# Four PSUM banks for the scores, and another order of work on the matrix engine, in a fused attention, MLP and routed-expert kernel

## The chip, the cores and the metric

The kernel runs as one program on one core of a Trainium2 chip. The metric is the device time of one execution in microseconds (us). The engines are TensorE (PE, matrix products; PEld is its weight load), VectorE (DVE), ScalarE (ACT), GpSimd (POOL) and SyncE (SP, which issues transfers). Each works through its own list of instructions in order; semaphores tie the lists together. PE writes its results into PSUM, eight banks of 512 float32 columns on 128 partitions.

## The reference

```python
# attention, per batch (4) and head (8): S = 576, D = 64
scores = q @ k.T / 8
kth    = the 32nd largest score of each row
attn   = softmax(where(scores >= kth, scores, -1e9))
x      = attn @ v                      # heads side by side: 2304 tokens x 512
# MLP: 512 -> 2048 -> 512
x = relu(x @ w_in) ** 2 @ w_out
# routed experts: 8 of 512 -> 1024 -> 512
compute = x @ w_skip > 0;  e = argmax(x @ w_gate);  g = softmax(x @ w_gate)[e]
out[compute] = x + g * (relu(x @ w1[e]) @ w2[e])
```

## The kernel before, in words

Attention runs in 72 steps (`NS`); step s takes 128 query rows of two heads (a "pair" step) or, in the middle group of eight, 64 left-over rows of four heads (a "mixed" step). Nine groups of eight steps (`GROUPS`, `PER_GROUP`) each fill 256 tokens of x; when a group is full, its MLP runs as 16 units (`FT`). A unit is `up` (12 matmuls of 256 columns) and `down` (6 matmuls of 512 columns) of the unit two places before. The engines' lists are written by one loop over t (`TIMES`). In iteration t the kernel does the scores of step t+1, the threshold and mask of t-1, the normalisation and transposes of t-2, the value product of t-3, and, from t = 10 (`FIRST`), two MLP units of an earlier group. So the MLP of group j fills PE while the attention of group j+1 goes on.

One step, by its names. `scores_half` (L1352, mixed L1358) multiplies q by one half of the keys, 288 columns for each of two heads. ACT copies each half to `s_sb` (`copy_scores`, L792). DVE pairs column i of the first half with column i of the second: `find_upper` (L1036) and `find_lower` (L1043) form the maxima and minima of all pairs, in one read from PSUM and in the other from `s_sb`. DVE then finds the 32nd largest with MAX8 and MATCH_REPLACE8 rounds (L1052, L1057, L1067, L1072), `pair_ranks` (L1083) and `find_kth` (L1090). POOL turns the result into two bias columns (`set_bounds`, L615 and L617), ACT computes a marker from them (`find_below`, L801, once for each head), POOL subtracts it (`mask`, L629), ACT exponentiates (L809), DVE inverts the sums (L1095) and POOL normalises (L623). PE transposes the probabilities (`transpose_probs`, L1377 and L1380), ACT copies them (`copy_transposed`, L816), PE multiplies by v (`values_product`, L1396), ACT copies the result twice (`copy_values`, L825 and L826) and POOL makes its low part (`split_x`, L635). In the MLP ACT does L834 and L843 and POOL L644 and L649 (`square_low`).

PSUM before: the scores' halves share banks 0 and 1, one after the other; the transposes use banks 2 to 4, the value product the rest of bank 4, `up` bank 5 and `down` banks 6 and 7. In three iterations of each group (`ENDS[j]`, +1, +2) PE also does the routing work on the finished group: `transpose_y` (L1449), `route_parts` (L1462) and `route` (L1473), in banks 2 and 3. After iteration 84 or so come the routed experts, about 150 us, which the change does not touch.

Unlike the order above, in the program PE's iteration before is: first half of the scores, value product, second half, transposes, unit, unit, routing. The rows of it stand in the next section but one.

Of the kernel before, what the change touches and what calls it, by code (L numbers as in the profile page):

```python
# [52 lines left out]
def build(nc, qT, kT, v_main, v_tail, w_in, w_out, w9, w1, w2, rows_scratch, out):  # L53
# [86 lines left out]
    with ExitStack() as ctx:  # L140
# [91 lines left out]
        def score_banks(s, half):  # L232


            at = 2 if s == 0 and half == 1 else 0
            return psum[:, at:at + 2, 0:HALF]

        pT_psum = psum_flat[:, 2 * 512:2 * 512 + PT_COLS]
        yT_psum = psum_flat[:, 2 * 512:4 * 512]
        values_psum = psum[:, 4, P:2 * P]  # L240
# [198 lines left out]
        def _(sp):  # L439
# [66 lines left out]
            for t in range(TIMES):  # L506
                for a in range(RING_A, len(LOADS_A)):
                    if FREED[a - RING_A] == t:
                        sp.wait_ge(scores_done, 2 * t + 2)
                        load_kq(a)  # L510
# [90 lines left out]
        def _(pool):  # L601
# [100 lines left out]
            for t in range(TIMES):  # L702
                slots = mlp_slots(t)
                if 0 <= t - 1 < NS:
                    set_bounds(t - 1)
# [3 lines left out]
                if 0 <= t - 3 < NS:  # L709
                    split_x(t - 3)  # L710
# [75 lines left out]
        def _(act):  # L786
            def copy_scores(s, half):
                act.wait_ge(scores_done, 2 * s + half + 1)
# [3 lines left out]
                nc.scalar.activation(s_sb[:, s % SBUFS, :, half * HALF:(half + 1) * HALF], score_banks(s, half), ACT.Copy,  # L792
# [19 lines left out]
            def copy_transposed(s):  # L812
                act.wait_ge(transposed, s + 1)
# [95 lines left out]
            copy_scores(0, 0)  # L909
            copy_scores(0, 1)  # L910
            for t in range(TIMES):
                slots = mlp_slots(t)
                if t + 1 < NS:
                    copy_scores(t + 1, 0)
                if 0 <= t - 1 < NS:
                    find_below(t - 1, 0)
                if 0 <= t - 3 < NS:
                    copy_values(t - 3)
                if t + 1 < NS:
                    copy_scores(t + 1, 1)  # L920
                if 0 <= t - 1 < NS:
                    find_below(t - 1, 1)
                for j in range(GROUPS):
                    if ENDS[j] == t:
                        copy_rows(j)
                if 0 <= t - 2 < NS:
                    copy_transposed(t - 2)
# [8 lines left out]
                for u in slots[0:1]:  # L936
                    square_high(u)
                if 0 <= t - 1 < NS:
                    exponentiate(t - 1, 1)
# [3 lines left out]
                for j in range(GROUPS):  # L943
                    if ENDS[j] == t:
                        copy_yT(j)
                    if ENDS[j] + 1 == t and j < GROUPS - 1:
                        copy_parts(j)
                    if ENDS[j] + 2 == t and j < GROUPS - 1:
                        copy_logits(j)
                if t == ENDS[GROUPS - 2] + 3:  # L950
# [76 lines left out]
        def _(dve):  # L1027
            v = nc.vector

            def find_upper(s):  # L1030


                dve.wait_ge(scores_copied, 2 * s + 2)

                wait(dve, upper_step, 14 * (s - 1))
                v.scalar_tensor_tensor(out=upper[:, s % 2, :, :], in0=score_banks(s, 1), scalar=SCALE,  # L1036
                                       in1=s_sb[:, s % SBUFS, :, 0:HALF], op0=ALU.mult, op1=ALU.max).then_inc(upper_set, 1)

            def find_lower(s):
# [3 lines left out]
                v.scalar_tensor_tensor(out=lower[:, s % 2, :, :], in0=score_banks(s, 1), scalar=SCALE,  # L1043
                                       in1=s_sb[:, s % SBUFS, :, 0:HALF], op0=ALU.mult, op1=ALU.min).then_inc(lower_set, 1)
# [289 lines left out]
        def _(pe):  # L1334
            t_ = nc.tensor

            def scores_half(s, half):
                kind, _, _, _, r, a = STEPS[s]
                if half == 0:
                    for x in range(a, a + (1 if kind == "pair" else 2)):  # L1340
                        pe.wait_ge(kq_loaded[x % RING_A], KQ_COUNT[x])

                if s > 0:
                    pe.wait_ge(scores_copied, 2 * s + half)
                if half == 0:
                    wait(pe, lower_set, s)
                banks = score_banks(s, half)
# [360 lines left out]
```

## Time and profile before

| | |
|---|---|
| median of 3 runs | 923.28 us (922.73 to 923.67) |
| the profiled execution: span from first to last instruction | 920.5 us |
| PE, PEld busy | 96%, 78% |
| DVE, ACT, POOL busy | 89%, 71%, 71% |
| mean granted TensorE clock | 0.985 of full |

The profiled execution has no time of its own beside the span; the runs around it are 2.2 to 3.2 us longer than the span, which is what lies outside the first and last instruction. A busy share counts an engine as busy while any of its instructions runs, and neighbouring instructions overlap at their ends. So the length of a stage is best read as the distance from its first start to the next stage's first start.

### The profile page before, as it was taken

To read this page: it belongs to the slowest core of one execution; us is meant where nothing else is said; L and a number is where in the kernel's file an instruction comes from. 1 tells how busy PE (TensorE), PEld (TensorE's weight loads), DVE (VectorE), ACT (ScalarE), POOL (GpSimd) and SP (SyncE) were. 2 spreads that over 40 slices of the span, in tenths; PEclk is the share of its full clock that TensorE was granted. 3 is DMA by queue.
4 is the path that set the end of the run, shared out by engine and by line. 5 is a ranking of instruction groups with operands and counts; after the bars stand their busy time and mean duration, and the time that the engine had idled before them with its cause. 6 is when DMAs were issued, how large, how long until landed. Compare 5 with 4: busy or idle time off the path is not lost.

```text
span 920.5 us, 21085 instructions
## 1 busy us (share of the span) xinstructions
PE 885.1 (96%) x6684; PEld 719.2 (78%) x6684; DVE 819.2 (89%) x2584; ACT 658.5 (72%) x1297; POOL 656.6 (71%) x884
## 2 busy tenths in 40 slices
PE   4799899999999999999999999999999999999997
PEld 2677687888888788888788887888878886788886
DVE  6999999999999999999999999999991064888887
ACT  3777787777777778777777777877775322788886
POOL 2999998878887787787888778778787452444432
PEclk7799999999999999999999999999999999999999
DMA  9962533566344658866535455433533675764990
GB/s 332 364 242 95 173 125 124 166 203 193 120 166 142 212 181 280 239 188 229 170 130 169 138 186 171 169 125 125 189 125 114 242 243 208 273 226 154 335 334 23
DMA packets 69750, 175.40 MB, mean 191 GB/s; under 512 B 21298, under 2 KB 26418, under 8 KB 65280
## 3 DMA queue, kind: packets, MB, share of 16 engines
q1 hardware_dynamic: 67568, 168.77, 54.2%
q0 software_dynamic: 1840, 5.06, 1.7%
q8 instruction: 56, 0.92, 0.4%
q14 instruction: 62, 0.51, 0.2%
q10 hardware_dynamic: 224, 0.15, 0.1%
HBM read 154.19 MB, written 21.27 MB: 191 GB/s over the span
## 4 chain that ended last, share of the span: by engine, by line
PE 84%; DVE 11%; POOL 2%; issue 1%; ACT 1%; DMA 0%; DVEq 0%; SPq 0%; POOLq 0%
PE psum L1352 8%; PE psum L1417 7%; PE psum L1418 7%; PE psum L1419 7%; PE psum L1377 7%; PE psum L1434 7%; PE psum L1435 7%; PE psum L1396 7%; PE psum L1436 7%; DVE top L1052 3%; DVE upper L1057 3%; PE psum L1650 2%; PE psum L1619 2%; PE psum L1624 2%; PE psum L1655 2%; PE psum L1658 2%
## 5 line engine op out<-in xcount | busy, mean ns | idle before, releaser
L1052 DVE MAX8 top<-upper 128x8 f32<-128x288 f32 x576 | 238.8, 446 | 0.0
L629 POOL TENSOR_TENSOR s_sb<-s_sb,below 128x576 f32<-128x576 f32 x144 | 203.3, 1434 | 1.5 <-ACT below L801 1.5
L1057 DVE MATCH_REPLACE8 upper<-top,upper 128x288 f32<-128x288 f32 x432 | 187.6, 441 | 0.0
L1417 PE MATMUL psum<-x_high,w_in_high 128*128 128x256 f32 x576 | 168.3, 292 | 1.6 <-POOL x_low L635 1.1
L1418 PE MATMUL psum<-x_low,w_in_high 128*128 128x256 f32 x576 | 161.8, 281 | 0.0
L1419 PE MATMUL psum<-x_high,w_in_low 128*128 128x256 f32 x576 | 161.2, 280 | 0.0
L792 ACT ACTIVATE s_sb<-psum 128x576 f32<-128x576 f32 x144 | 93.8, 651 | 93.7 <-PE psum L1352 84.2
L644 POOL TENSOR_TENSOR square<-relu 128x256 f32<-128x256 f32 x144 | 89.7, 623 | 81.7 <-ACT relu L834 80.9
L649 POOL TENSOR_TENSOR g_low<-square,g_high 128x256 fp32r<-128x256 f32 x144 | 108.4, 753 | 30.3 <-POOL square L644 23.2
L1352 PE MATMUL psum<-k_sb,q_sb 64*128 64x288 f32 x512 | 100.1, 469 | 21.7 <-DVE lower L1043 19.1
L801 ACT ACTIVATE below<-s_sb,steep_kth 128x576 f32<-128x576 f32 x144 | 110.8, 770 | 9.2 <-POOL neg_max L617 8.4
L1067 DVE MAX8 top<-lower 128x8 f32<-128x288 f32 x288 | 115.3, 441 | 0.0
L1434 PE MATMUL psum<-w_ring,g_high 128*128 128x512 f32 x288 | 114.5, 398 | 0.0
L1435 PE MATMUL psum<-w_ring,g_high 128*128 128x512 f32 x288 | 113.5, 394 | 0.0
L1436 PE MATMUL psum<-w_ring,g_low 128*128 128x512 f32 x288 | 113.2, 393 | 0.0
L1417 PEld LDWEIGHTS psum<-x_high,w_in_high 128*128 128x128 f32 x576 | 108.5, 188 | 6.0 <-POOL x_low L635 1.3
L1418 PEld LDWEIGHTS psum<-x_low,w_in_high 128*128 128x128 f32 x576 | 108.7, 189 | 3.2
L809 ACT ACTIVATE s_sb<-s_sb,neg_max 128x576 f32<-128x576 f32 x144 | 110.9, 770 | 0.0
L834 ACT ACTIVATE relu<-psum 128x256 f32<-128x256 f32 x144 | 55.5, 385 | 76.1 <-PE psum L1419 75.0
L1419 PEld LDWEIGHTS psum<-x_high,w_in_low 128*128 128x128 f32 x576 | 108.6, 189 | 0.0
L623 POOL TENSOR_SCALAR s_sb<-s_sb,sums 128x576 f32<-128x576 f32 x144 | 106.3, 749 | 0.0
L1377 PEld LDWEIGHTS psum<-ident,s_sb 128*128 128x128 f32 x576 | 62.1, 142 | 34.0 <-issue 30.2
(213 smaller groups left out, 1848.0 us busy)
## 6 DMA issues: line engine op xcount, KB each, us to landing
w_ring<-w_split SPq DMA_DIRECT2D x144, 512.0 KB, 4.5
weights<-w SPq DMA_DIRECT2D x32, 1024.0 KB, 7.1
v_sb<-v_main SPq DMA_DIRECT2D x48, 256.0 KB, 2.5
w_split<-w_ring SPq DMA_DIRECT2D x16, 512.0 KB, 4.3
k_sb<-kT SPq DMA_DIRECT2D x32, 144.0 KB, 4.5
k_sb<-kT SPq DMA_DIRECT2D x32, 128.0 KB, 4.3
weights<-w_out SPq DMA_DIRECT2D x1, 4096.0 KB, 13.5
weights<-w_in SPq DMA_DIRECT2D x1, 4096.0 KB, 21.1
```

Source lines behind the costliest of these rows:

```text
L629: nc.gpsimd.tensor_tensor(s_sb[:, s % SBUFS, n, 0:S], s_sb[:, s % SBUFS, n, 0:S], below[:, n, :], ALU.subtract).then_inc(masked, 1)
L1052: v.max(top[:, s % 2, n, 8 * r:8 * r + 8], upper[:, s % 2, n, :]).then_inc(upper_step, 1)
L1057: v.match_replace(upper[:, s % 2, n, :], top[:, s % 2, n, 8 * r:8 * r + 8], upper[:, s % 2, n, :], LOWEST).then_inc(upper_step, 1)
L1067: v.max(top[:, s % 2, n, at:at + 8], lower[:, s % 2, n, :]).then_inc(lower_step, 1)
L1352: last = t_.matmul(banks[:, n, :], q_sb[own, a % RING_A, r * P:(r + 1) * P], k_sb[own, a % RING_A, cols], start=True, stop=True)
L1377: t_.transpose(psum[:, 2 + n, k * P:(k + 1) * P], tiles[:, at:at + P], ident[:, :])
L1417: t_.matmul(dst, wh, x_high[:, j % 2, k, :], start=k == 0, stop=False)
L1418: t_.matmul(dst, wh, x_low[:, j % 2, k, :], start=False, stop=False)
L1419: last = t_.matmul(dst, wl, x_high[:, j % 2, k, :], start=False, stop=k == KC - 1)
L1434: t_.matmul(psum[:, 6 + c, :], gh, wh, start=f == 0, stop=False)
L1435: t_.matmul(psum[:, 6 + c, :], gh, wl, start=False, stop=False)
L1436: last = t_.matmul(psum[:, 6 + c, :], gl, wh, start=False, stop=f == FT - 1)
```

## The change

The two halves of the scores get banks of their own: the first half banks 0 and 1, the second banks 2 and 3. The second half shares its banks with the transposes and the routing work, so each of these waits for the other's copy. The scores of a step are now done in one piece and copied by ACT with one instruction over four banks (128x1152). DVE's pair passes read the first half from PSUM and the second from `s_sb`. PE's iteration becomes: scores, unit, transposes of t-2, unit, routing, value product of t-2 (no longer t-3). ACT and POOL follow that order: `copy_values` and `split_x` come first in the iteration, both `find_below` come before the scores' copy, and `copy_transposed` comes after the first exponential. The first unit of a group may start its first chunks of k before the last low part of x is there.

On PE, an iteration in the middle of the program (`U` and `D` of the text are the L1417 to L1419 and the L1434 to L1436 matmuls), before:

```order
L1352 MATMUL psum<-k_sb,q_sb 128x288 x2
L1396 MATMUL psum<-pT_sb,v_sb 64x128 x8
L1396 MATMUL psum<-pT_sb,v_last 64x128 x2
L1352 MATMUL psum<-k_sb,q_sb 128x288 x2
L1377 MATMUL psum<-ident,s_sb 128x128 x8
L1380 MATMUL psum<-ident,s_sb 128x128
L1417 MATMUL psum<-x_high,w_in_high 128x256
```

The same place after, from the value product on (L1411 is the value product, L1350 the scores, L1437 to L1439 and L1454 to L1456 a unit, L1394 and L1395 the transposes; the dots leave out repeats inside a unit):

```order
L1411 MATMUL psum<-pT_sb,v_sb 64x128 x8
L1411 MATMUL psum<-pT_sb,v_last 64x128 x2
L1350 MATMUL psum<-k_sb,q_sb 128x288 x4
L1437 MATMUL psum<-x_high,w_in_high 128x256
...
L1456 MATMUL psum<-w_ring,g_low 128x512
L1394 MATMUL psum<-ident,s_sb 128x128 x8
L1395 MATMUL psum<-ident,s_sb 128x128
L1437 MATMUL psum<-x_high,w_in_high 128x256
```

The two pieces of scores have become one, a unit stands between them and the transposes, and the value product has moved from between the scores' halves to the end of the iteration.

On ACT, one iteration before:

```order
L792 ACTIVATE s_sb<-psum 128x2x288
L801 ACTIVATE below<-s_sb,steep_kth 128x576
L825 ACTIVATE x_now<-psum 128x128
L826 ACTIVATE x_high<-psum 128x128
L792 ACTIVATE s_sb<-psum 128x2x288
L801 ACTIVATE below<-s_sb,steep_kth 128x576
L816 ACTIVATE pT_sb<-psum 128x1152
L834 ACTIVATE relu<-psum 128x256
L809 ACTIVATE s_sb,sums<-s_sb,neg_max 128x576
L843 ACTIVATE g_high<-relu 128x256
```

and after (L833 and L834 copy the values, L807 is `find_below`, L791 the scores' copy, L842 and L851 the unit's, L815 the exponential, L824 the transposes' copy):

```order
L833 ACTIVATE x_now<-psum 128x128
L834 ACTIVATE x_high<-psum 128x128
L807 ACTIVATE below<-s_sb,steep_kth 128x576 x2
L791 ACTIVATE s_sb<-psum 128x1152
L842 ACTIVATE relu<-psum 128x256
L815 ACTIVATE s_sb,sums<-s_sb,neg_max 128x576
L851 ACTIVATE g_high<-relu 128x256
L824 ACTIVATE pT_sb<-psum 128x1152
```

The scores' copy now stands behind both `find_below`, which wait for POOL's bounds of step t-1.

The diff, cut to what the prediction speaks of:

```diff
         @block.gpsimd: for t in range(TIMES):
+                if 0 <= t - 3 < NS:
+                    split_x(t - 3)
                 if 0 <= t - 1 < NS:
                     set_bounds(t - 1)
                 if 0 <= t - 2 < NS:
                     normalise(t - 2, 0)
                     normalise(t - 2, 1)
-                if 0 <= t - 3 < NS:
-                    split_x(t - 3)
...
+            def copy_scores(s):
+                act.wait_ge(scores_done, s + 2)
                 if s >= SBUFS:
                     act.wait_ge(transposed, s - SBUFS + 1)
+                nc.scalar.activation(s_sb[:, s % SBUFS, :, :].rearrange("p n (h c) -> p n h c", h=2),
+                                     psum[:, 0:4, 0:HALF].rearrange("p (h n) c -> p n h c", h=2), ACT.Copy,
+                                     scale=SCALE).then_inc(scores_copied, 1)
...
             def find_upper(s):
-                dve.wait_ge(scores_copied, 2 * s + 2)
+                dve.wait_ge(scores_copied, s + 2)
                 wait(dve, upper_step, 14 * (s - 1))
-                v.scalar_tensor_tensor(out=upper[:, s % 2, :, :], in0=score_banks(s, 1), scalar=SCALE,
-                                       in1=s_sb[:, s % SBUFS, :, 0:HALF], op0=ALU.mult, op1=ALU.max).then_inc(upper_set, 1)
+                v.scalar_tensor_tensor(out=upper[:, s % 2, :, :], in0=score_banks(0), scalar=SCALE,
+                                       in1=s_sb[:, s % SBUFS, :, HALF:S], op0=ALU.mult, op1=ALU.max).then_inc(upper_set, 1)
...
+            def scores(s):
...
+                if s > 0:
+                    pe.wait_ge(scores_copied, s + 1)
+                wait(pe, lower_set, s)
+                last = scores_half(s, 0)
...
+                wait(pe, transposed_copied, s - 3)
...
+                scores_half(s, 1).then_inc(scores_done, 1)
 
             def transpose_probs(s):
+                pe.wait_ge(scores_copied, min(s + 3, NS - 1) + 2)
                 wait(pe, transposed_copied, s)
+                wait(pe, values_copied, s)
...
             def up(u):
+                whole = KC - 1 if ORDER[j] else KC - 2
                 if f == 0:
-                    pe.wait_ge(x_low_done, PER_GROUP * (j + 1))
+                    pe.wait_ge(x_low_done, PER_GROUP * (j + 1) - (2 if ORDER[j] else 1))
...
                 for k in range(KC):
+                    if f == 0 and k == whole:
+                        pe.wait_ge(x_low_done, PER_GROUP * (j + 1))
...
             for t in range(TIMES):
                 if t + 1 < NS:
-                    scores_half(t + 1, 0)
-                if 0 <= t - 3 < NS:
-                    values_product(t - 3)
-                if t + 1 < NS:
-                    scores_half(t + 1, 1)
-                if 0 <= t - 2 < NS:
-                    transpose_probs(t - 2)
+                    scores(t + 1)
                 if 2 <= t < FIRST:
                     keep_clock(20)
+                if not slots and 0 <= t - 2 < NS:
+                    transpose_probs(t - 2)
                 for u in slots:
                     up(u)
                     down(u - DOWN_LAG)
...
+                    if u % 2 == 0 and 0 <= t - 2 < NS:
+                        transpose_probs(t - 2)
+                routing_share(t)
+                if 0 <= t - 2 < NS:
+                    values_product(t - 2)
```

`routing_share(t)` holds the calls of `transpose_y`, `route_parts` and `route` that stood at the iteration's end before. `copy_rows` moves from the start of iteration `ENDS[j]` to the end of the one before it.

## Rows read from the trace of the kernel before

**Rows 1.** The page: busy us, share of the span and instructions of each engine.

```profile
PE 885.1 (96%) x6684; PEld 719.2 (78%) x6684; DVE 819.2 (89%) x2584; ACT 658.5 (72%) x1297; POOL 656.6 (71%) x884
```

**Rows 2.** Timeline, PE, one ordinary step: start us, us, instructions merged.

```profile
244.86 0.76 PE L1352 MATMUL psum<-k_sb,q_sb 64*128 64x288 f32 x4
245.54 1.09 PE L1396 MATMUL psum<-pT_sb,v_sb 128*64 128x128 f32 x16
...
246.78 0.76 PE L1352 MATMUL psum<-k_sb,q_sb 64*128 64x288 f32 x4
247.47 1.09 PE L1377 MATMUL psum<-ident,s_sb 128*128 128x128 f32 x8
...
248.43 0.36 PE L1417 MATMUL psum<-x_high,w_in_high 128*128 128x256 f32 x1
...
249.93 0.39 PE L1434 MATMUL psum<-w_ring,g_high 128*128 128x512 f32 x1
...
252.74 0.39 PE L1434 MATMUL psum<-w_ring,g_high 128*128 128x512 f32 x1
...
254.22 0.51 PE L1352 MATMUL psum<-k_sb,q_sb 64*128 64x288 f32 x2
```

**Rows 3.** Timeline, PE: four iterations later, three of them with routing work.

```profile
263.60 0.76 PE L1352 MATMUL psum<-k_sb,q_sb 64*128 64x288 f32 x4
...
303.04 0.71 PE L1358 MATMUL psum<-k_sb,q_mixed 64*64 64x288 f32 x8
```

**Rows 4.** Timeline, DVE: ends of search 56.62, 65.95, 243.91; then one pair pass.

```profile
56.62 0.16 DVE L1090 TENSOR_REDUCE kth<-mins 128x2 f32<-128x34 f32 x1
...
65.95 0.16 DVE L1090 TENSOR_REDUCE kth<-mins 128x2 f32<-128x34 f32 x1
...
243.91 0.17 DVE L1090 TENSOR_REDUCE kth<-mins 128x2 f32<-128x34 f32 x1
...
250.30 0.75 DVE L1036 SCALAR_TENSOR_TENSOR upper<-psum,s_sb 128x576 f32<-128x576 f32 x1
```

**Rows 5.** Timeline, PE, the first scores of the program.

```profile
4.38 2.01 PE L1352 MATMUL psum<-k_sb,q_sb 64*128 64x288 f32 x8 [0.30 <-DMA k_sb<-kT]
...
10.19 1.33 PE L1352 MATMUL psum<-k_sb,q_sb 64*128 64x288 f32 x4 [0.74 <-ACT s_sb L792]
```

**Rows 6.** Timeline, ACT, in the step of rows 2.

```profile
246.90 0.28 ACT L825 ACTIVATE x_now<-psum 128x128 f32<-128x128 f32 x1
247.08 0.27 ACT L826 ACTIVATE x_high<-psum 128x128 fp32r<-128x128 f32 x1
...
248.13 0.77 ACT L801 ACTIVATE below<-s_sb,steep_kth 128x576 f32<-128x576 f32 x1
248.80 1.13 ACT L816 ACTIVATE pT_sb<-psum 128x1152 f32<-128x1152 f32 x1
```

**Rows 7.** Timeline, POOL, in the same step.

```profile
244.73 0.73 POOL L649 TENSOR_TENSOR g_low<-square,g_high 128x256 fp32r<-128x256 f32 x1
245.43 0.20 POOL L615 TENSOR_SCALAR steep_kth<-kth 128x2 f32<-128x2 f32 x1
245.59 0.19 POOL L617 TENSOR_SCALAR neg_max<-top 128x2 f32<-128x2 f32 x1
...
247.43 0.46 POOL L635 TENSOR_TENSOR x_low<-x_now,x_high 128x128 fp32r<-128x128 f32 x1 [0.20 <-ACT x_high L826]
247.85 1.43 POOL L629 TENSOR_TENSOR s_sb<-s_sb,below 128x576 f32<-128x576 f32 x1
```

**Rows 8.** Timeline, POOL, near 27 us.

```profile
25.70 2.49 POOL L657 TENSOR_TENSOR w_ring<-weights,w_ring 128x512 fp32r<-128x512 f32 x2
```

**Rows 9.** Timeline, DVE, at the same time.

```profile
27.21 1.03 DVE L1083 TENSOR_TENSOR mins<-top 128x34 f32<-128x34 f32 x1
```

**Rows 10.** Timeline, PE, after the last scores.

```profile
689.54 0.63 PE L1377 MATMUL psum<-ident,s_sb 128*128 128x128 f32 x4 [0.49 <-POOL s_sb L623]
...
716.07 0.39 PE L1417 MATMUL psum<-x_high,w_in_high 128*128 128x256 f32 x1 [1.08 <-POOL x_low L635]
```

More of the change, by code:

```diff
@@ L942, in _ @@
                     square_high(u)
-                for j in range(GROUPS):
+                for j in range(GROUPS - 1):
                     if ENDS[j] == t:
                         copy_yT(j)
-                    if ENDS[j] + 1 == t and j < GROUPS - 1:
+                    if ENDS[j] + 1 == t:
                         copy_parts(j)
-                    if ENDS[j] + 2 == t and j < GROUPS - 1:
+                    if ENDS[j] + 2 == t:
                         copy_logits(j)
+                for j in range(GROUPS):
+                    if ENDS[j] - 1 == t:
+                        copy_rows(j)
+                if t == ENDS[GROUPS - 1]:
+                    copy_yT(GROUPS - 1)
                 if t == ENDS[GROUPS - 2] + 3:
@@ L1338, in scores_half @@
                 kind, _, _, _, r, a = STEPS[s]
[L1339 to L1347, printed above, removed]
                 cols = slice(half * HALF, (half + 1) * HALF)
@@ L1351, in scores_half @@
                         own = slice(n * HD, (n + 1) * HD)
-                        last = t_.matmul(banks[:, n, :], q_sb[own, a % RING_A, r * P:(r + 1) * P],
+                        last = t_.matmul(psum[:, 2 * half + n, 0:HALF], q_sb[own, a % RING_A, r * P:(r + 1) * P],
                                          k_sb[own, a % RING_A, cols], start=True, stop=True)
@@ L1513, in _, with routing_share @@
             keep_clock(5)
-            scores_half(0, 0)
-            scores_half(0, 1)
+            def routing_share(t):
+                for j in range(GROUPS - 1):
+                    if ENDS[j] == t:
+                        transpose_y(j)
+                    if ENDS[j] + 1 == t:
+                        route_parts(j)
+                    if ENDS[j] + 2 == t:
+                        route(j)
+            scores(0)
             for t in range(TIMES):
@@ L1542, in _ @@
                     up_ahead(0, [0])
-                for j in range(GROUPS):
-                    if ENDS[j] == t:
-                        transpose_y(j)
-                    if ENDS[j] + 1 == t and j < GROUPS - 1:
-                        route_parts(j)
-                    if ENDS[j] + 2 == t and j < GROUPS - 1:
-                        route(j)
+                    transpose_y(GROUPS - 1)
                 if t == ENDS[GROUPS - 1] + 1:
```

69 lines of the change are left out of this document (33 added, 36 removed).

## The prediction

> **What bounds the kernel now.** I read the page first: PE is busy 96% of the span and DVE 89%, ACT and POOL 71% each [rows 1]. In the attention part PE and DVE are both busy without a break, so busy shares can't tell which sets the pace. The timeline can, by the distance from one step's start to the next.
>
> DVE alone: before the MLP has begun, when PE has room, its search ends come 65.95 - 56.62 = 9.33 us apart [rows 4]. That is DVE's own pace.
>
> PE alone, one ordinary step, start to start [rows 2]: scores half 0.68 (244.86 to 245.54), value product 1.24, scores half 0.69, transposes 0.96, first `up` 1.50, `down`, `up` 2.81, second `down` 1.48. The sum is 9.36, no stage among them has an idle time in the timeline, so PE works back to back, a hair slower than DVE. With routing work four steps take 303.04 - 263.60 = 39.44 [rows 3], which is 4 x 9.36 + 2.0. So a group of eight costs PE 8 x 9.36 + 2.0 = 76.9 and DVE only 8 x 9.33 = 74.6. PE sets the pace, with DVE 2.3 us per group behind it. The reader is to see that a PE step made shorter by more than some 0.3 us brings nothing more.
>
> **What PE saves in a step.** The counts of matmuls stay. What goes is one change between kinds of product. A lone half lasts 0.69, although its columns account for less: the nine transposes of 128 columns take 0.96 [rows 2], 0.107 each, so 288 columns are 0.24, and a half is two of these in each of two row groups that run side by side, 0.48. The 0.2 left is filling and emptying. Joined, a half is to cost 0.48 more, not 0.69 more: 0.69 + 0.48 = 1.17. Bounds for the joined piece: above 1.37, two lone halves; below, eight instructions took 2.01 where four took 1.33 at the low clock [rows 5], a ratio of 1.51, and 1.51 x 0.69 = 1.04 (the clock rose during the eight, so this is too low). I take 1.17, near the column count.
>
> The other changes of kind in the new order: scores to `up` is not in the trace; transposes to `up` costs the unit 1.50 against 1.42 (2.81 less a `down` of 1.39), so I take 1.50, bounds 1.42 and 1.60 (what a half loses altogether). Value product to scores 1.24 as now. `down` to value product 1.48, as `down` to scores now. `down` to transposes and routing: 1.39, and the transposes then lack part of their fill, 0.92 (0.90 to 0.96). The step becomes 1.24 + 1.17 + 1.50 + 1.39 + 0.92 + 1.50 + 1.48 = 9.20, or 0.16 less. A group becomes 8 x 9.20 + 2.0 = 75.6, 1.3 less, and PE still sets the pace, 1.0 above DVE. Over the 62 iterations that hold both attention and units (t = 10 to 71) PE saves 62 x 0.16 = 9.9. In the first nine of them, before any routing, DVE's 9.33 holds PE back, so 9 x 0.13 = 1.2 of it is not had. First term: -9.
>
> The Trainium skill weighs the same place by a rule: "Changing tiling mode (not just tile) drains the TensorE" (TensorEngine Tiling (Array Packing), Tiling Modes). Scores use 64-row tiles, values 64-column ones, all else the full array. By the rule four changes of mode in a step become three, and what is saved is one drain and no column time. With the whole 0.2 of a half as the drain the rule gives the same 9.2. The step of rows 2 shows the loss at each such change but cannot show whether scores to `up` costs as much as scores to transposes.
>
> **What the copies cost.** ACT copied two halves of 0.65; now it copies 1152 columns at once. The trace has that size: 1.13 [rows 6], which is contiguous where the new one is in four pieces. ACT's total falls by a tenth, and ACT isn't the bound. What counts is where the copy stands. Before, the second half's copy had only one L801 ahead; now both stand ahead, and they wait for POOL's bounds, which stand behind `split_x`, which waits for the value product. And the transposes now wait for the copy. That makes a loop through PE:
>
> value product ends; to ACT 0.1; `copy_values` 0.45 (246.90 to 247.35) [rows 6]; to POOL 0.08; `split_x` 0.42 (247.43 to 247.85); L615 and L617 0.35 (245.43 to 245.78) [rows 7]; to ACT 0.03; two L801 at 0.68 (248.13 to 248.80), 1.35; the copy 1.13 [rows 6]; to PE 0.05. Together 3.96 from the value product to the transposes. PE itself gets there by scores, `up`, `down`: 1.17 + 1.50 + 1.39 = 4.06. So the transposes find the copy done 0.1 us before, and the loop costs nothing; behind the waiting transposes stand the unit, routing and value product of the iteration, so any wait would lengthen the step in full. Cost taken: 0, with bounds of 0 and 0.07 per step, for a copy between 1.13 and 1.30 (two halves of 0.65). In iterations with routing PE's part of the loop grows by the same work as PE's step, so the 0.1 stays.
>
> DVE needs the copy 6.2 us after its own `find_kth` ended (243.91 + 0.17 to 250.30) [rows 4]; the way there is 0.1 + 0.35 + 0.03 + 1.35 + 1.13 = 3.0. DVE isn't kept waiting. The waits for the previous transposes' copy and for `copy_rows`, moved on ACT, are for work that ended a whole unit (2.8) earlier. SP's loads hang on the same counts as before, and the v slots are freed an iteration earlier for a product that comes nearly an iteration earlier; the lead stays over a step. No cost.
>
> **After the last scores.** There PE waits for POOL before the transposes (0.49 for the first head, about 0.2 for the second, in two steps, and half that in a third) and 1.08 for the last low part of x [rows 10]. After, a unit (2.8 us) stands ahead of the transposes and covers the first; the last value product is an iteration earlier and the first unit's leading chunks cover the second. Together 0.7 + 0.7 + 0.4 + 1.1 = 2.9, of which nothing else on PE takes the place. Second term: -3.
>
> **The sum.** 920.5 - 9 - 3 = 908.5 as a span. The runs are a median of 2.8 above the span, so 911.3 against 923.28.
>
> **Rivals.**
>
> The first: DVE's pace holds. If joined scores come near 1.04 and `up` loses nothing, PE's group falls to DVE's 74.6. The attention steps then gain (76.9 - 74.6) per group over 7.75 groups, 17.8, less the first nine steps' share of about 3, and 3 behind: about 906. For it: rows 5. Against: that ratio spans a rise of the clock. Chance 0.13.
>
> The second: half of it goes in new losses on PE. The joined scores stay nearer 1.37 less 0.1, or leaving them costs `up` 0.1 more: saved 0.06 to 0.08 a step, 5 us, plus 3: 916. Chance 0.10, and 0.05 for the end of this case in which nothing is left, 923.
>
> The third: POOL holds DVE up. L1083 took 1.03 us where it takes 0.17, and it ended with POOL's L657 (25.70 + 2.49 = 28.19 against 27.21 + 1.03 = 28.24) [rows 8, 9]. So this one DVE instruction, which reads two SBUF operands, can wait for a POOL instruction to end. The order moves POOL's work against DVE's. Where L1083 falls is between PE's scores and 5.6 us behind their end, as DVE leads or lags; POOL's masks of 1.43 [rows 7] run some 1.9 to 4.7 us behind that end while DVE is already a search further, so it can meet L644 or L649 (0.73) at the unit's end but hardly a mask. A mean hold of 0.13 us per step is hidden by PE's 75.6 against DVE's 74.6; 0.3 gives 8 x 9.63 = 77.0, no gain in the steps. Middle: 0.2, 76.2 per group, gain 5.4 + 3, 915. Chance 0.05.
> The Trainium skill has this as a rule: a DVE instruction with two SBUF inputs and a GpSimd instruction that reads SBUF lock each other out of a shared port for the whole instruction (SBUF — State Buffer, Who interferes with whom). The trace agrees, by the pair of rows at 27 us.
>
> The fourth, slower: the loop through the copy becomes the bound. It has 0.1 us to spare. The place is the transposes' wait for `scores_copied`. If the four-piece copy, or ACT's turn behind POOL, takes 0.5 longer than the rows add up to, each step is 9.20 + 0.4 = 9.60, a group 78.8, 1.9 more than before, over 7.75 groups +15, less 3 behind: 935. It decides from 0.1 and turns the sign from about 0.3. For it: five hand-overs between engines in series, none of which had slack in my sum. Against: each piece is a row. Chance 0.08.
>
> **How the numbers follow.** The forecast has 0.59, the rivals 0.13, 0.10, 0.05, 0.05 (915) and 0.08. Faster by over 0.2% (1.8 us, about what a measurement of this kernel tells from no change): 0.59 + 0.13 + 0.10 + 0.05 = 0.87, less 0.01: 0.86. Within: 0.05. Slower: 0.09. The range leaves out the slower case and "no change" above, and goes down to the DVE case: 904.5 to 919. The forecast's own range is 908 to 914, from the bounds of the joined scores (0.05 either way makes 3).
>
> **What would show it.** L1350 x4 spans about 1.17 to the first L1437; ordinary steps of 9.2 to 9.35 on PE; DVE's search ends 9.33 apart in ordinary steps; transposes (L1394) with no idle time ahead of them, from `scores_copied` above all; `pair_ranks` (L1090 now) staying at 0.17 to 0.2; no wait of 1.08 at the last group's first unit. The prediction is wrong if the transposes wait for the copy in most steps, if joined scores last over 1.3, or if DVE's step exceeds 9.5.

## The result, and the profile after

The changed kernel takes 912.55 us (median of 4 runs, 911.1 to 913.32). The kernel before took 923.16 us beside it (922.73 to 923.67). The ratio is 0.9885, with a 95% interval of 0.9871 to 0.9899. The prediction was 911.3, with a range of 904.5 to 919.

The profiled execution after has a span of 910.6 us, 9.9 less than before. In every run on record with a span listed, the time is 1.7 to 1.9 us above that run's own span. So the 2.2 to 3.2 us between the times and the 920.5 of the kernel before are not all time outside the first and last instruction: its profiled execution was itself about 1 us faster than the median. That is why the spans differ by 9.9 and the medians by 10.6. The TensorE clock is no rival here. The profiled execution before had a mean granted clock of 0.985, the one after 0.999. But other runs of the kernel before with 0.998 or more take 922.5 to 923.1 us, and those with 0.985 and 0.986 take 922.0 and 922.2.

First the page, in answer to [rows 1]:

```profile
PE 872.4 (96%) x6684; PEld 724.1 (80%) x6684; DVE 821.0 (90%) x2584; ACT 645.1 (71%) x1226; POOL 656.1 (72%) x884
```

The shares hardly changed. The gain shows in the distance between steps. (PE's matmuls and the weight loads, PEld, are listed apart.) The timeline of PE over one ordinary step answers to [rows 2] (start us, us, instructions merged; repeats inside a unit are left out):

```profile
462.85 1.24 PE L1350 MATMUL psum<-k_sb,q_sb 64*128 64x288 f32 x8
464.02 0.39 PE L1437 MATMUL psum<-x_high,w_in_high 128*128 128x256 f32 x1
...
465.56 0.39 PE L1454 MATMUL psum<-w_ring,g_high 128*128 128x512 f32 x1
...
466.95 1.03 PE L1394 MATMUL psum<-ident,s_sb 128*128 128x128 f32 x8
...
467.85 0.36 PE L1437 MATMUL psum<-x_high,w_in_high 128*128 128x256 f32 x1
...
469.36 0.39 PE L1454 MATMUL psum<-w_ring,g_high 128*128 128x512 f32 x1
...
470.86 1.09 PE L1411 MATMUL psum<-pT_sb,v_sb 128*64 128x128 f32 x16
```

From start to start: scores 1.17, `up` 1.54, `down` 1.39, transposes 0.90, `up` 1.51, `down` 1.50, and the value product 1.24 as before. That is 9.25, and 9.24 on average in ordinary steps. A group of eight, from one scores' start to that eight steps on, takes 75.7 (414.9 to 490.6). It was 76.9. In such a group PE and DVE both have no idle time now. The stretches below are one group before and one after (us; busy time of PE, PEld, DVE, ACT, POOL; then granted clock, DMA share and GB/s):

```profile
427.92:504.84 76.92, 76.92 (x605) 62.72 (x604) 75.23 (x266) 58.59 (x125) 61.44 (x89) 1.00 0.51 159
```

```profile
425.04:500.71 75.67, 75.67 (x606) 63.36 (x604) 75.67 (x267) 57.21 (x117) 61.49 (x88) 1.00 0.53 164
```

What DVE's 1.1 us beyond its own 74.6 consist of is told under the port below.

The loop through the copy, in the same steps (timeline of ACT, PE and POOL):

```profile
465.65 1.12 ACT L791 ACTIVATE s_sb<-psum 128x1152 f32<-128x1152 f32 x1
466.95 1.03 PE L1394 MATMUL psum<-ident,s_sb 128*128 128x128 f32 x8
470.86 1.09 PE L1411 MATMUL psum<-pT_sb,v_sb 128*64 128x128 f32 x16
...
472.22 0.28 ACT L833 ACTIVATE x_now<-psum 128x128 f32<-128x128 f32 x1 [1.39 <-PE psum L1411]
472.39 0.27 ACT L834 ACTIVATE x_high<-psum 128x128 fp32r<-128x128 f32 x1
472.74 0.46 POOL L633 TENSOR_TENSOR x_low<-x_now,x_high 128x128 fp32r<-128x128 f32 x1 [0.84 <-ACT x_high L834]
473.17 0.19 POOL L613 TENSOR_SCALAR steep_kth<-kth 128x2 f32<-128x2 f32 x1
473.32 0.20 POOL L615 TENSOR_SCALAR neg_max<-top 128x2 f32<-128x2 f32 x1
473.55 1.44 ACT L807 ACTIVATE below<-s_sb,steep_kth 128x576 f32<-128x576 f32 x2 [0.89 <-POOL neg_max L615]
474.90 1.11 ACT L791 ACTIVATE s_sb<-psum 128x1152 f32<-128x1152 f32 x1
```

The value product gives way to the next scores at 470.86 + 1.24 = 472.10. The copy ends at 474.90 + 1.11 = 476.01, and 0.05 more hands it to PE: 3.96. The transposes start 4.10 behind the scores' start (462.85 to 466.95). So 0.14 is to spare for the matmuls, and the loop does not set the pace here. Their weight load (PEld) has no such room: it starts at 466.82, just behind the end of the copy at 465.65 + 1.12 = 466.77.

Early on, before any routing work, DVE's 9.33 is slower than PE's 9.24. There the transposes do wait a little for the copy, which PE can afford: it is not the engine that sets the pace there. The same rows near 133 us:

```profile
134.72 1.11 ACT L791 ACTIVATE s_sb<-psum 128x1152 f32<-128x1152 f32 x1
135.88 0.86 PEld L1394 LDWEIGHTS psum<-ident,s_sb 128*128 128x128 f32 x8 [0.37 <-ACT s_sb L791]
```

Behind the last scores, PE has no idle time ahead of its transposes at 691.70, where [rows 10] had 0.49, nor ahead of the last group's first unit, where they had 1.08. But one new wait has come up at the very end of the units (timeline of ACT and PE after):

```profile
757.65 0.60 ACT L879 ACTIVATE rows<-psum 128x512 f32<-128x512 f32 x1 [3.79 <-PE psum L1456]
758.15 0.59 ACT L961 ACTIVATE ahead_xT<-psum 128x512 f32<-128x512 f32 x1
758.79 1.12 PE L1519 MATMUL psum<-weights,ahead_xT 128*128 128x512 f32 x2 [1.18 <-ACT ahead_xT L961]
```

The same place before:

```profile
767.35 0.60 ACT L954 ACTIVATE ahead_xT<-psum 128x512 f32<-128x512 f32 x1 [2.40 <-PE psum L1535]
...
768.54 1.02 PE L1499 MATMUL psum<-weights,ahead_xT 128*128 128x512 f32 x2
...
768.74 0.60 ACT L871 ACTIVATE rows<-psum 128x512 f32<-128x512 f32 x1 [0.79 <-PE psum L1436]
```

Before, ACT copied `ahead_xT` while PE was still on its last `down`. The change put `copy_rows` of the last group ahead of it in ACT's queue. That copy needs the last `down`, so `ahead_xT` now comes late. (The idle times of 2.40 and 3.79 are ACT's own.)

The 9.9 us by stretches, from the two profiled executions: up to the end of the last scores -8.3 (681.0 to 672.7). From there to the end of the last `down` -2.8 (87.7 to 84.9). Behind it +1.2 (151.8 to 153.0).

### The profile page after: what moved, and what is told of

Its sections match the earlier page's. It is cut to its first block, busy times and chain, and to the rows that moved or that the text cites. A ratio compares the mean times of both kernels' runs of the same rounds, so it can differ in the third digit from the quotient of the medians.

```text
span 910.6 us, 21039 instructions
## 1 busy us (share of the span) xinstructions
PE 872.4 (96%) x6684; PEld 724.1 (80%) x6684; DVE 821.0 (90%) x2584; ACT 645.1 (71%) x1226; POOL 656.1 (72%) x884
## 4 chain that ended last, share of the span: by engine, by line
PE 86%; DVE 12%; issue 1%; ACT 1%; DMA 0%; POOL 0%; SPq 0%; DVEq 0%
PE psum L1437 9%; PE psum L1411 8%; PE psum L1438 7%; PE psum L1439 7%; PE psum L1455 7%; PE psum L1454 7%; PE psum L1456 7%; PE psum L1350 7%; PE psum L1394 6%; DVE top L1059 3%; DVE upper L1064 3%; PE psum L1674 2%; PE psum L1643 2%; PE psum L1648 2%; PE psum L1679 2%; PE psum L1652 2%
## 5 line engine op out<-in xcount | busy, mean ns | idle before, releaser
L1437 PE MATMUL psum<-x_high,w_in_high 128*128 128x256 f32 x576 | 174.6, 303 | 0.0
L1439 PE MATMUL psum<-x_high,w_in_low 128*128 128x256 f32 x576 | 161.8, 281 | 0.0
L807 ACT ACTIVATE below<-s_sb,steep_kth 128x576 f32<-128x576 f32 x144 | 104.0, 769 | 75.4 <-POOL neg_max L615 75.4
L1437 PEld LDWEIGHTS psum<-x_high,w_in_high 128*128 128x128 f32 x576 | 108.5, 188 | 25.6 <-issue 21.9
L815 ACT ACTIVATE s_sb<-s_sb,neg_max 128x576 f32<-128x576 f32 x144 | 110.8, 769 | 9.3 <-POOL s_sb L627 2.2
L647 POOL TENSOR_TENSOR g_low<-square,g_high 128x256 fp32r<-128x256 f32 x144 | 108.6, 754 | 11.3
L1454 PE MATMUL psum<-w_ring,g_high 128*128 128x512 f32 x288 | 113.9, 396 | 0.0
L1456 PE MATMUL psum<-w_ring,g_low 128*128 128x512 f32 x288 | 113.9, 395 | 0.0
L1439 PEld LDWEIGHTS psum<-x_high,w_in_low 128*128 128x128 f32 x576 | 108.6, 189 | 0.0
L1350 PE MATMUL psum<-k_sb,q_sb 64*128 64x288 f32 x512 | 83.6, 447 | 16.1 <-DVE lower L1050 15.5
L824 ACT ACTIVATE pT_sb<-psum 128x1152 f32<-128x1152 f32 x72 | 80.4, 1116 | 8.6 <-PE psum L1395 8.6
L633 POOL TENSOR_TENSOR x_low<-x_now,x_high 128x128 fp32r<-128x128 f32 x72 | 32.8, 456 | 68.5 <-ACT x_high L834 68.5
L791 ACT ACTIVATE s_sb<-psum 128x1152 f32<-128x1152 f32 x71 | 78.9, 1112 | 3.9 <-PE psum L1350 3.9
```

Of the source, the lines that this page charges most:

```text
L815: nc.scalar.activation(tile, tile, ACT.Exp, bias=neg_max[:, s % 2, n:n + 1], accum_out=sums[:, s % 2, n:n + 1]).then_inc(exp_done, 1)
L1350: last = t_.matmul(psum[:, 2 * half + n, 0:HALF], q_sb[own, a % RING_A, r * P:(r + 1) * P], k_sb[own, a % RING_A, cols], start=True, stop= ...
L1437: t_.matmul(dst, wh, x_high[:, j % 2, k, :], start=k == 0, stop=False)
L1439: last = t_.matmul(dst, wl, x_high[:, j % 2, k, :], start=False, stop=k == KC - 1)
L1454: t_.matmul(psum[:, 6 + c, :], gh, wh, start=f == 0, stop=False)
L1456: last = t_.matmul(psum[:, 6 + c, :], gl, wh, start=False, stop=f == FT - 1)
```

## The experiments

### The copy of `ahead_xT` first

```diff
+                if t == ENDS[GROUPS - 1] - 1:
+                    act.wait_ge(ahead_transposed, 1)
+                    nc.scalar.activation(ahead_xT[:, :], psum[:, 4, :], ACT.Copy).then_inc(ahead_xT_done, 1)
                 for j in range(GROUPS):
                     if ENDS[j] - 1 == t:
                         copy_rows(j)
...
-                if t == ENDS[GROUPS - 1] - 1:
-                    act.wait_ge(ahead_transposed, 1)
-                    nc.scalar.activation(ahead_xT[:, :], psum[:, 4, :], ACT.Copy).then_inc(ahead_xT_done, 1)
```

> ScalarE copies the ahead rows (ahead_xT) before copy_rows of the last group instead of behind it. Theory: in the changed kernel PE stood idle for 1.18 us at the first up_ahead, because ahead_xT was queued on ACT behind a copy that waits for the last down product. Then the wait goes, the last down product is followed by up_ahead at once, and the time falls by 1.2 us, 912.55 to 911.4. Rival: the next thing behind it (the last rows' copies, the transposed rows, the search for the experts' places on VectorE) is late anyway and the time stays within 0.3 us.

Measured: 911.28 us (910.81 to 911.36), 1.3 less than the changed kernel's 912.55, with a ratio to before of 0.9878 (0.9861 to 0.9894). The times alone do not settle it. The kernel before took 922.58 beside this run and 923.16 beside the changed kernel, and the intervals of the two ratios overlap. The trace does: the wait is gone, and PE goes straight on at 757.65:

```profile
756.45 0.60 ACT L954 ACTIVATE ahead_xT<-psum 128x512 f32<-128x512 f32 x1 [2.40 <-PE psum L1560]
...
757.65 1.02 PE L1519 MATMUL psum<-weights,ahead_xT 128*128 128x512 f32 x2
```

From the last `down` to the end it is 151.7, as before the change (151.8), where the changed kernel has 153.0. That microsecond has its cause.

### Scores in two pieces again

```diff
             scores(0)
+            scores_rest(0)
...
+                if 0 <= t - 3 < NS:
+                    values_product(t - 3)
+                if t + 1 < NS:
+                    scores_rest(t + 1)
...
-                if 0 <= t - 2 < NS:
-                    values_product(t - 2)
```

> The value product stands between the two halves of the scores again; banks, ACT's single copy and all other orders stay as changed. Theory: what a step gained is one filling and emptying of the array between kinds of product, 0.20 us. Scores then last 0.69 + 0.69 around the value product, an ordinary step 9.24 + 0.20 = 9.44, and with 55 steps at PE's pace and the first ten at VectorE's the time rises by 10 to 12 us, to about 923, all of the gain. Rival: the gain came from the order of transposes and units (what covers what), and joining is worth little: under 3 us more.

Measured: 952.13 us (950.44 to 954.08), ratio 1.0318 (1.0298 to 1.0338). That is 40 us above the changed kernel, not some 11. The step is 9.85, within rounding of scores 0.69, values 1.24, scores 0.69, `up` 1.52, `down` 1.76, transposes 0.95, `up` 1.51, `down` 1.50. Of the 0.6 over 9.24, 0.21 is the price of two lone halves (0.69 + 0.69 against 1.17). The rest is a wait that I had not put in the sum (timeline of PE, ACT and POOL):

```profile
470.98 0.76 PE L1350 MATMUL psum<-k_sb,q_sb 64*128 64x288 f32 x4
...
471.10 0.28 ACT L833 ACTIVATE x_now<-psum 128x128 f32<-128x128 f32 x1 [1.75 <-PE psum L1413]
...
473.78 1.11 ACT L791 ACTIVATE s_sb<-psum 128x1152 f32<-128x1152 f32 x1
...
474.95 0.44 PE L1396 MATMUL psum<-ident,s_sb 128*128 128x128 f32 x2 [0.20 <-ACT s_sb L791]
```

The value product ends at 470.98, and the transposes start 3.97 later. That is the same loop again. But with only half of the scores behind the value product, PE's own way is 0.69 + 1.52 + 1.40 = 3.61, so PE waits 0.36 in every ordinary step (the 0.20 in the row is only the part that the profile puts down to this release). Only the 0.48 us of scores that joining put behind the value product keep the loop, which the prediction called harmless, from ruling the kernel. Joining saves 0.2 of scores directly, and it is also what makes the copy's place on ACT affordable.

### A longer loop

```diff
+                wait(act, pad_written, s - 1)
+                nc.scalar.activation(pad[:, :, :], ident[:, :].unsqueeze(1).to_broadcast([P, 3, P]),
+                                     ACT.Copy).then_inc(pad_written, 1)
                 nc.scalar.activation(s_sb[:, s % SBUFS, :, :].rearrange("p n (h c) -> p n h c", h=2),
```

> One more ScalarE copy of 384 columns (about 0.4 us from start to next start) stands ahead of the scores' copy in each step; its result is not used. Theory: the loop value product, values' copy, low part, bounds, two markers, scores' copy, transposes has 0.13 us to spare against PE's own way, so PE waits 0.27 us ahead of the transposes in each step, 9.24 becomes 9.5 and the time rises by 15 us (12 to 18), to 927. Rival: ACT is only 71% busy, so 0.4 us more per step costs nothing; or the loop has no slack at all, and it costs 0.4 x 60 = 24.

Measured: 933.71 us (933.26 to 934.49), ratio 1.0121 (1.0104 to 1.0138), which is 21 above the changed kernel and outside the 12 to 18 expected. The timeline of ACT and PE:

```profile
470.31 0.51 ACT L790 ACTIVATE pad<-ident 128x384 f32<-128x384 f32 x1
470.73 1.11 ACT L795 ACTIVATE s_sb<-psum 128x1152 f32<-128x1152 f32 x1
471.89 0.85 PEld L1399 LDWEIGHTS psum<-ident,s_sb 128*128 128x128 f32 x8 [0.56 <-ACT s_sb L795]
```

The added copy moves the next by 470.73 - 470.31 = 0.42. Less the 0.14 to spare that is 0.28. The step grew by 0.34 (9.24 to 9.58); the other 0.06 is the transposes' weight load, which no longer runs ahead (0.96 for the transposes instead of 0.90). Up to the last scores the kernel lost 21.7 us: 1.7 in the first iterations, before there are units, and 20.0 in the 60 steps after, 0.33 each. So the expectation missed the weight load and the first iterations. Of its rivals, "costs nothing" falls; "no slack at all" (24) comes near in the time, but the 0.28 of the timeline speaks for the slack of 0.14. The prediction's fourth rival was a true mechanism at about the price it stated, and it stood 0.14 us away.

### The transposes right behind the scores

```diff
-                if not slots and 0 <= t - 2 < NS:
+                if 0 <= t - 2 < NS:
                     transpose_probs(t - 2)
...
-                    if u % 2 == 0 and 0 <= t - 2 < NS:
-                        transpose_probs(t - 2)
```

> In every step with units the transposes stand right behind the scores, ahead of both units, with everything else as in the changed kernel. Theory: the loop from the end of the values through their copy, the splitting of x, the bounds, both counts and the copy of the scores to the transposes takes 3.96 us, of which only the scores' 1.17 lies in TensorE's way: TensorE waits 2.8 us in each of some 62 steps, the step is 9.24 + 2.8 = 12.0 us and the whole near 912.6 + 62 x 2.8 = 1085 (1060 to 1110). Rival: the loop is not tied to the end of the values but to VectorE's pace, and the transposes wait only till VectorE's bounds are copied: a step of 9.3 to 9.8 and 915 to 950.

Measured, one run: 1177.17 us, worse than the theory's 1085. The wait is as computed (timeline of PE):

```profile
484.17 1.20 PE L1356 MATMUL psum<-k_sb,q_mixed 64*64 64x288 f32 x16
488.13 1.40 PE L1394 MATMUL psum<-ident,s_sb 128*128 128x128 f32 x8 [2.76 <-ACT s_sb L791]
```

3.96 from the scores' start to the transposes: the loop, to the hundredth. But a step takes 13.54, not 12.0. The same kernel by stretches (busy us of each engine; the 0.76, 0.50, 0.97 are the granted clock):

```profile
484.00:488.00 4.00, 1.37 (x25) 0.61 (x20) 4.00 (x16) 2.83 (x5) 3.19 (x6) 1.00 0.44 134
488.10:489.40 1.30, 1.27 (x10) 1.28 (x10) 1.30 (x6) 0.00 (x0) 1.30 (x2) 0.76 1.11 415
489.40:492.10 2.70, 2.70 (x14) 2.70 (x13) 1.84 (x4) 0.00 (x0) 0.37 (x1) 0.50 0.98 237
492.10:493.50 1.40, 1.40 (x7) 1.17 (x7) 0.00 (x0) 1.16 (x4) 0.62 (x1) 0.97 1.02 223
```

In the stretch behind the idle 2.76 us PE has only half of its clock, 1.2 GHz, for one whole `up`: 2.71 instead of 1.52. The transposes take 1.26 instead of 0.90. So 9.24 + 2.76 + 1.19 + 0.36 = 13.55. Three steps of the same run give the comparison (starts at 155.62, 292.09 and 401.37). The wait is the same, but the granted clock stays at 1.00, and each takes 11.96, the 12.0 of the theory:

```profile
159.58 1.09 PE L1394 MATMUL psum<-ident,s_sb 128*128 128x128 f32 x8 [2.72 <-ACT s_sb L791]
```

So the 1.5 us beyond the wait are the clock's, and in most steps of this kernel the wait is paid for one and a half times. This is why the change needs both parts. The scores' copy is not there before 3.96, and the unit that now stands in between fills that time.

### The tail in its old order

```diff
-                whole = KC - 1 if ORDER[j] else KC - 2
+                whole = 0 if j == GROUPS - 1 else KC - 1 if ORDER[j] else KC - 2
...
-                if not slots and 0 <= t - 2 < NS:
+                if (not slots or t >= NS) and 0 <= t - 2 < NS:
                     transpose_probs(t - 2)
```

> The steps behind the last scores go back to the order of the kernel before (transposes ahead of the units), and the last group's first unit waits for all of x_low at once. Theory: the waits for probabilities and for x_low that are seen in the tail of the kernel before (0.7, 0.7, 0.4 and 1.1) come back, nothing else changes: 912.6 + 2.9 = 915.5 (914.6 to 916.0). Rival: the tail was shortened by the joined scores and by the state in which the last search leaves the queues, not by the order: 912.6.

Measured: 919.58 us (917.99 to 920.65), ratio 0.9964 (0.995 to 0.9978). That is +7.0, where +2.9 was expected. All of it lies behind the last scores: these start at the same time (672.4 against 672.3), and the last `down` ends at 763.7 against 757.6. The waits are back, in the two steps whose order was turned back, but longer (2.51 and 1.89), with 1.17 for `x_low`. In the timeline of PE:

```profile
691.44 1.30 PE L1394 MATMUL psum<-ident,s_sb 128*128 128x128 f32 x8 [2.51 <-POOL s_sb L621]
```

where [rows 10] had 0.49. The likely reason is the rest of the change: on POOL `split_x` now stands ahead of the bounds and of `normalise`, and on ACT the second exponential stands behind the transposes' copy. In the trace `normalise` starts at 690.55, behind a `split_x` that had waited for the value product. No run turned these orders back one by one in the tail. The probabilities of a step come 1.4 to 2.0 us later in PE's order than they did. So the rival (no effect) falls, and the unit ahead of the transposes is worth 6 to 7 us, not 2.9. Some 3 to 4 of these pay for waits that the change itself would have made. The net of the tail is the -2.8 of the ledger.

### `split_x` back behind `normalise`

```diff
-                if 0 <= t - 3 < NS:
-                    split_x(t - 3)
                 if 0 <= t - 1 < NS:
                     set_bounds(t - 1)
                 if 0 <= t - 2 < NS:
                     normalise(t - 2, 0)
                     normalise(t - 2, 1)
+                if 0 <= t - 3 < NS:
+                    split_x(t - 3)
```

> GpSimd's order as in the kernel before: bounds and both normalisations first, then the low part of x. The loop through the scores' copy then is shorter by the 0.42 us of the low part and by its wait for the value product. Theory: PE sets the pace in nearly all of the attention part, the loop does not, so the time stays within 1 us of 912.5; the copy of the scores ends 0.4 or more earlier ahead of the transposes. Rival: the loop sets the pace, and the time falls by 0.4 us per step, some 20 us in all, until VectorE's 9.33 stops it (about 906).

Measured: 914.87 us (914.45 to 915.88), ratio 0.9921 (0.9904 to 0.9938), 2.3 more than the changed kernel and outside what was expected. PE's own steps stayed at 9.24, although the scores' copy starts 1.8 instead of 2.8 us behind the value product in them. So the loop does not set the pace, and this rival falls. About half of the loss lies in the DVE-paced stretch. There four search ends in a row stand 9.79 apart, three of them 0.4 more than in the changed kernel (ends of DVE's search, L1097, here):

```profile
123.25 0.17 DVE L1097 TENSOR_REDUCE kth<-mins 128x2 f32<-128x34 f32 x1
133.05 0.17 DVE L1097 TENSOR_REDUCE kth<-mins 128x2 f32<-128x34 f32 x1
142.84 0.16 DVE L1097 TENSOR_REDUCE kth<-mins 128x2 f32<-128x34 f32 x1
```

In the changed kernel the same search ends are 123.33, 132.73 and 142.11. In this kernel `pair_ranks` (L1090) takes 0.65 at 132.12. POOL's L647 runs there from 131.98 for 0.73, to 132.71:

```profile
131.98 0.73 POOL L647 TENSOR_TENSOR g_low<-square,g_high 128x256 fp32r<-128x256 f32 x1
```

0.65 - 0.18 = 0.47 is what each such step is longer than 9.33. The Trainium skill's rule on the shared port (SBUF — State Buffer, Who interferes with whom), that a DVE instruction with two SBUF inputs and a GpSimd instruction that reads SBUF lock each other out, was cited at the prediction's third rival. The trace agrees: the DVE instruction ends within 0.06 us of POOL's, and where DVE sets the pace the hold is paid in full.

These steps cost 1.2 us. The other half is a wait that the theory had left out. The low part of x comes later now, and the first unit of a group waits for it on PE:

```profile
182.68 0.19 PEld L1437 LDWEIGHTS psum<-x_high,w_in_high 128*128 128x128 f32 x1 [1.19 <-POOL x_low L633]
```

This step is 1.2 us longer than in the changed kernel, and one near 334 us is 0.4 longer in the same way. Against these stand 0.5 gained in the first iterations, which differ by 0.4 between the changed kernel and the first experiment too, although these do the same there.

### PE made lighter

```diff
-                    t_.matmul(dst, wh, x_low[:, j % 2, k, :], start=False, stop=False)
-                    last = t_.matmul(dst, wl, x_high[:, j % 2, k, :], start=False, stop=k == KC - 1)
+                    last = t_.matmul(dst, wh, x_low[:, j % 2, k, :], start=False, stop=k == KC - 1)
+                    if k < KC - 1:
+                        last = t_.matmul(dst, wl, x_high[:, j % 2, k, :], start=False, stop=False)
```

> This kernel leaves out one of the twelve matmuls of every up product (low half of the weights times high half of x, for the last k), so that TensorE's step is lighter and VectorE's pace is laid bare. A unit's up product of 12 matmuls takes 1.51, so one matmul is 0.126 and two units make a step 0.25 shorter: TensorE alone would need 9.24 - 0.25 = 8.99 us, below VectorE's 9.33. Theory: VectorE sets the pace at 9.33 in the ordinary steps; a group of 8 steps is 74.6 instead of 75.7, and the waits of the pair minima for the port with GpSimd, 6.9 us over the run and harmless so far, now count in part: 7.3 groups at -1.1 is -8, the up products of the units outside the ordinary steps and of the tail some -1 to -2, and +2 to +5 from the port: 907 (905 to 909). Rival: GpSimd's and ScalarE's chain of the bounds holds VectorE at the present pace: the gain is only that of the tail, 911.

Measured: 904.3 us (903.36 to 905.87), ratio 0.98 (0.9784 to 0.9817), 8.2 less than the changed kernel and 0.7 below the range given. Of the 8.1 by which the spans differ, 6.3 lie ahead of the last scores and 1.9 between them and the last `down`. DVE sets the pace: its search ends are 9.33 apart in ordinary steps and a group takes 74.8. The +2 to +5 for the port did not come. `pair_ranks` is held for 1.9 us in all 72 steps, where the changed kernel has 6.9. So the holds are a matter of how DVE and POOL stand to each other: in this kernel they hardly meet. That group times fell from 75.7 to 74.8 also shows that PE, and not DVE with its holds, set the pace of the changed kernel.

### Both orders on ACT mended

```diff
-                if 0 <= t - 2 < NS:
+                if t >= FIRST and 0 <= t - 2 < NS:
                     copy_transposed(t - 2)
                 if 0 <= t - 1 < NS:
                     exponentiate(t - 1, 1)
+                if t < FIRST and 0 <= t - 2 < NS:
+                    copy_transposed(t - 2)
```

The edit of the first experiment is in it too.

> Two orders on ScalarE are mended in the changed kernel. The copy of ahead_xT goes ahead of the last group's row copy (alone it gave 911.28 against 912.55), and in the steps that have no units the copy of the transposed tiles goes behind the second exponential. Theory: VectorE's reciprocal of the row sums waited 0.9 us for that exponential in step 2, which made the 20th search end 1.0 us later than before; the whole is 912.6 - 1.2 - 1.0 = 910.3 (909.7 to 910.9), and the 20th search ends near 197.1. Rival: the microsecond at the start is taken up by another wait before TensorE sets the pace, so it gives nothing: 911.3.

Measured: 910.98 us (910.04 to 911.29), ratio 0.9869 (0.9852 to 0.9885). It is faster than the kernel before. Its span (908.9) is 1.7 below the changed kernel's, while the intervals of the two ratios still overlap. From the first experiment's 911.28 it is 0.3 away, within the spread. The theory of the start mostly fell: the 20th search ends at 197.65, not 197.1, where the changed kernel has 198.07 and the first experiment 198.38. DVE's wait of 0.94 for the exponential is gone, and in the next step this took its place (timeline of DVE, and then of POOL):

```profile
46.38 0.90 DVE L1092 TENSOR_TENSOR mins<-top 128x34 f32<-128x34 f32 x1
```

```profile
44.70 2.53 POOL L655 TENSOR_TENSOR w_ring<-weights,w_ring 128x512 fp32r<-128x512 f32 x2
```

44.70 + 2.53 = 47.23 and 46.38 + 0.90 = 47.28: the hold of [rows 8, 9] once more, 0.72 long. The kernel before had it too, two steps earlier. The rival (another wait takes up the start's microsecond) was right for most of it.

## Why the prediction was right, and where it was not

**The step of PE: right.** Joined scores 1.17, as taken; the step 9.24, where 9.20 was given. The small misses: the first `up` 1.52 to 1.54 for 1.50, `down` ahead of the value product 1.50 for 1.48, transposes 0.90 for 0.92. A group takes 75.7 for 75.6, but here two misses cancel: eight steps are 0.3 longer than forecast, and the routing work adds 1.8, not 2.0. The first and second rival fall by this: PE stayed above DVE's 74.6, and hardly anything was lost again. The first rival's support was misread, too. The granted clock is 1.00 during the eight matmuls of [rows 5] and 0.50 during the four, so their ratio, and the lower bound of 1.04 worked out from it, say nothing. That a lone half wastes 0.2 is shown directly by the pieces of the second experiment.

**The first term, -9: right in size, -8.3 up to the last scores.** It holds a part that I had not seen. The 20th search ends 0.9 later than before (198.07 against 197.14). Of this 0.5 comes with the very first search (first search end 18.9 for 18.4). Steps 10 to 13 give +0.6, since `pair_ranks` is held up there by POOL. The 0.94 wait for ACT in step 2 stands against a like hold before. The other differences cancel. The part that PE paces then gained 7.6 between the 20th and the last search, and the last scores gained more than the last search, which now lies 1.7 further behind them. What the 0.5 of the first search depends on was not tried. About 0.3 of such a difference is spread: in this kernel and in two others that do the same up to there (the first and the fifth experiment), the 20th search ends between 198.07 and 198.38.

**The copy, 0: right, and by as little as stated.** 0.1 was given as the slack and 0.14 was there. The experiments give the price on the other side: 0.42 more in the loop costs 21 us, and 0.48 less of PE work beside it, with the lone halves, costs 40. The fourth rival was not wrong in mechanism; only its condition did not come about.

**The second term, -3: right in sum, -2.8, and partly for another reason.** I took the waits of [rows 10] as what the new order saves. With the other engines in their new order those waits would have been 5.6 us (2.51, 1.89 and 1.17), and the tail 6.0 longer. The cover was worth more, and it also covered what the change made late.

**The step that failed: "The waits for the previous transposes' copy and for `copy_rows`, moved on ACT, are for work that ended a whole unit (2.8) earlier."** For `copy_rows` it holds in no group. In the first seven the copy starts right as the `down` it waits for ends, with ACT idle for 0.07 to 0.14, and nothing on PE waits for it. In the eighth ACT idles 0.55, as it did before the change. In the last one that `down` is the last of all, ACT idles 3.79, and behind the copy stood the one of `ahead_xT`, for which PE waited 1.18. With this order mended the kernel took 911.28.

**The sum: near, and in part by luck.** In spans the forecast was -12 and the result -9.9. The missing 2.1 are 1.2 for `ahead_xT`, 0.7 of the first term and 0.2 of the second. The time came within 1.3 us of 911.3 all the same, because the 2.8 us added to the span held 1.0 by which the profiled execution before was faster than its median.

**The port, nothing: right for the time, wrong for the row.** I had said that `pair_ranks` would stay at 0.17 to 0.2. Its median did (0.176), but it went up to 0.707, and the holds grew from 1.7 to 6.9 us. They are free as long as PE sets the pace, but they fill DVE's room. From the 21st search on, every distance between search ends but one is 9.33 plus the hold in it, within 0.04 (9.75 with 0.41, 9.55 with 0.22). The holds come to 1.0 us in a group, of the 1.1 that DVE had to spare. So they take up what DVE would else have idled. Whether more holds would then cost time was not tried.

## What to carry to other kernels

Before work is put in front of a copy in a queue, add up the whole loop from the producer through every hand-over back to it, and compare it with what the waiting engine has to do meanwhile. Here that was 3.96 against 4.10, and each tenth beyond would have cost 6 to 7 us (an estimate from 62 steps, and from the 20 us that 0.28 cost). A large piece of gapless work on the engine that sets the pace (here a whole unit) belongs in front of the instruction with the longest supply chain, not behind it. Look at the last iteration by itself: an order that is harmless in all others may put a wait for the very last result in front of something that was ready.

## What the runs showed of the hardware

- A visit to the scores (64-row tiles) costs about 0.2 on top of its columns, once per visit: one half takes 0.69 alone, and two in one go 1.17.
- One ACT instruction that copies 1152 columns out of four separate banks takes 1112 ns on average (71 of them). A copy of 1152 columns without gaps takes 1116. The four pieces cost nothing here.
- An idle time of 2.76 us on PE was followed by a stretch at the lower of its two clocks (0.50 granted), and the first `up` took 2.71 instead of 1.52. In three steps of the same run an idle time of 2.72 to 2.75 was followed by no such fall. Idle times of 0.2 to 0.35 in every step of the second and third experiment came with a granted clock of 1.00 in the stretches read, and an `up` of 1.51.
- A DVE instruction of two SBUF operands that normally takes 0.17 lasted until POOL's running instruction was over, within 0.06: 0.90 beside L655, 0.65 beside L647.
